# Attention output stored without its normalisation and scaled at the first expert layer's input; the products with V grouped, the near scores put between them

## The reference

```python
q_rot, k_rot = rotate(q), rotate(k)                       # q, k, v: (4, 8, 576, 64), float32
scores = (1 / sqrt(64)) * q_rot @ k_rot.T
scores = scores - max(scores, axis=-1)
attn = exp(scores)
attn = attn / (sum(attn, axis=-1) + 1e-09)
x = attn @ v                                              # rearranged to (2304 tokens, 512)
h = x @ w_in1;  x = (h - tanh(h)) @ w_out1                # w_in (512, 2048), w_out (2048, 512)
h = x @ w_in2;  out = (h * sigmoid(1.702 * h)) @ w_out2
```

## Time and profile before

| | |
|---|---|
| runs, median | 1148.81 us |
| profiled execution | 1147.27 us, of which the span is 1145.5 us |
| PE busy | 1104.1 us, 96% |
| DVE busy | 552.4 us, 48% |
| ACT busy | 425.7 us, 37% |
| POOL busy | 57.1 us, 5% |
| R of head 0, R of head 31 | at 23.05 us, at 325.15 us |
| first expert matmul | at 337.05 us |

### The profile page before, as it was taken

How to read it: one execution, slowest core, us unless ns; L and a number is a source line. 1 busy time by engine, 2 the same in 40 slices (tenths; PEclk the granted TensorE clock), 3 DMA queues, 4 the chain that set the end, 5 groups by cost and what they waited for, 6 DMA issues and landing times.

```text
span 1145.5 us, 15078 instructions
## 1 busy us (share of the span) xinstructions
PE 1104.1 (96%) x5952; PEld 1017.8 (89%) x5952; DVE 552.4 (48%) x879; ACT 425.7 (37%) x747; POOL 57.1 (5%) x62
## 2 busy tenths in 40 slices
PE   2999998999999999999999999999999999999998
PEld 1888877787789999999999999999999999999997
DVE  7888887888736433232233333455232322323222
ACT  2555554555544423222222323445232222323222
POOL 3011111102111000000000000000000000000000
PEclk9999999999999999999999999999999999999999
DMA  6355557566315300000000100062000000000000
GB/s 182 95 158 127 155 154 201 136 169 166 87 61 178 102 28 29 28 28 11 19 28 28 29 28 28 1 193 83 28 28 28 28 1 28 28 28 1 28 1 28
DMA packets 78854, 79.85 MB, mean 70 GB/s; under 512 B 30144, under 2 KB 55744, under 8 KB 78784
## 3 DMA queue, kind: packets, MB, share of 16 engines
q1 hardware_dynamic: 78784, 78.89, 24.1%
HBM read 55.12 MB, written 14.23 MB: 61 GB/s over the span
## 4 chain that ended last, share of the span: by engine, by line
PE 89%; DVE 7%; SPq 1%; DMA 1%; POOL 1%; issue 1%; ACT 0%; POOLq 0%; DVEq 0%; ACTq 0%
PE PS L485 35%; PE PS L503 17%; PE PS L500 17%; PE PS L449 10%; PE PS L414 3%; PE PS L431 3%; PE PS L437 3%; DVE neg_max L667 2%; DVE q_max L684 1%; DVE k_hl L679 1%; DVE q_max L674 1%; DMA turned_k<-k_dram 1%; DVE raw_q L662 0%; DVE w_parts L697 0%; DVE raw_q L660 0%
## 5 line engine op out<-in xcount | busy, mean ns | idle before, releaser
L485 PE MATMUL PS<-x_hi,w_parts 128*128 128x384 f32 x1536 | 423.1, 336 | 0.0
L742 DVE TENSOR_TENSOR g_raw<-PS,act_t 128x384 f32<-128x384 f32 x192 | 107.0, 557 | 400.2 <-ACT act_t L610 202.1
L485 PEld LDWEIGHTS PS<-x_hi,w_parts 128*128 128x128 f32 x1536 | 280.5, 188 | 4.3
L485 PE MATMUL PS<-x_lo,w_parts 128*128 128x384 f32 x768 | 257.2, 335 | 0.0
L500 PE MATMUL PS<-g_hi,w_parts 128*128 128x384 f32 x768 | 210.3, 334 | 0.8 <-DVE g_lo L747 0.8
L503 PE MATMUL PS<-w_parts,g_hi 128*128 128x512 f32 x576 | 195.1, 393 | 1.0 <-DVE y_sb L756 0.8
L449 PE MATMUL PS<-probs,v_one 128*128 128x288 f32 x640 | 183.4, 409 | 0.3 <-ACT pv_sb L545 0.3
L747 DVE TENSOR_TENSOR g_lo<-g_raw,g_hi 128x384 fp32r<-128x384 f32 x192 | 107.7, 561 | 113.6 <-ACT g_hi L617 113.6
L537 ACT ACTIVATE probs<-PS 128x576 f32<-128x576 f32 x160 | 104.0, 650 | 129.6 <-PE PS L437 126.3
L485 PEld LDWEIGHTS PS<-x_lo,w_parts 128*128 128x128 f32 x768 | 144.2, 188 | 4.2
L617 ACT ACTIVATE g_hi<-g_raw 128x384 fp32r<-128x384 f32 x192 | 100.8, 525 | 122.9 <-DVE g_raw L742 119.7
(11 more groups left out here) (51 smaller groups left out, 741.3 us busy)
## 6 DMA issues: line engine op xcount, KB each, us to landing
x_raw<-x_scratch SPq DMA_DIRECT2D x12, 768.0 KB, 4.5
raw_w<-moe_w_in_dram SPq DMA_DIRECT2D x32, 256.0 KB, 3.1
raw_w<-moe_w_out_dram SPq DMA_DIRECT2D x32, 256.0 KB, 3.3
raw_k<-k_dram SPq DMA_DIRECT2D x16, 288.0 KB, 3.5
turned_k<-k_dram SPq DMA_DIRECT2D x64, 72.0 KB, 3.2
raw_q<-q_dram SPq DMA_DIRECT2D x16, 288.0 KB, 3.8
turned_q<-q_dram SPq DMA_DIRECT2D x64, 72.0 KB, 3.5
k_one<-k_hl SPq DMA_DIRECT2D x32, 144.0 KB, 2.4
```

The lines of the kernel that those rows point to most:

```text
L485: last = nc.tensor.matmul(h_banks[j % 2], w_parts[j][:, w, c * P:(c + 1) * P], x[par][:, c, :], start=(c == 0 and w == 0 and x is x_hi), s ...
L742: nc.vector.tensor_tensor(g_raw[:, j % 2, :], h_banks[j % 2], act_t[:, j % 2, :], ALU.subtract if m == 0 else ALU.mult).then_inc(g_done, 1)
```

## The change

Three edits, made together.

1. `pv_sb` goes to `x_scratch` as it is, one DMA a head, from SP right behind that head's sums. The inverses go to `inv_scratch`, laid out as x is. `load_x` of the first layer fetches, beside x, the inverses of the unit in two DMAs that repeat each row over 64 partitions, into the new tile `inverses`. DVE multiplies x by them (`scale_x`, four instructions of 128x384 a unit) ahead of `cut_x`, and ACT's part of `cut_x` waits for each. `spread_inverse`, `normalise` and POOL's `tile_mask` are gone. In iterations 17 and 19, ACT's part of `cut_x` is now behind the exponential of tile 4 in place of tile 2.
2. `place_maxima` is moved from DVE to ACT: five copies of 5x128 instead of one DVE instruction of 5x640, each with a column of the identity as its per-partition scale, behind the exponential of tile 2.
3. The order of PE and with it `RING`: PV comes in groups of two, one and two, and the near scores of tiles 1 to 4 stand singly or in a pair around them.

```diff
-PV_LAG = 2
+NEAR_BEFORE = {0: (1,), 1: (4,)}
+NEAR_AFTER = {0: (2, 3)}
...
             def store_inverse(pair):
+                row, col = pair % PAIRS_PER_BATCH, pair // PAIRS_PER_BATCH * SEQ
...
-            def spread_inverse(pair):
...
-            def store_x(pair):
...
+            def store_x(h):
+                pair, a = h // 2, h % 2
+                row, col = pair % PAIRS_PER_BATCH * P + a * HD, pair // PAIRS_PER_BATCH * SEQ
+                sp.wait_ge(pv_copied, h + 1)
+                sp.dma_start(x_scratch[0][row:row + HD, col:col + SEQ], pv_sb[h % 4][own(a), :]).then_inc(x_stored[h % 4], 16)
...  load_x
+                if m == 0:
+                    for j in range(2):
+                        sp.wait_ge(inv_out[j], 16 * batches * PAIRS_PER_BATCH // 2)
+                    if u:
+                        sp.wait_ge(x_scaled, u * KC)
+                    for a in range(2):
+                        rows = inv_scratch.rearrange("c a n -> a c n")[a:a + 1, :, u * UNIT:(u + 1) * UNIT]
+                        sp.dma_start(inverses[own(a), :, :], rows.broadcast_to([HD, KC, UNIT])).then_inc(inverses_in, 16)
...  POOL
-            nc.gpsimd.memset(tile_mask, 0.0).then_inc(pool_chain, 1)
...
-            def normalise(pair):
...
-                for a in range(2):
-                    last = nc.gpsimd.tensor_tensor(x_out[par][own(a), :], pv_sb[(2 * pair + a) % 4][own(a), :],
-                                                   inv_wide[par][own(a), :], ALU.mult)
...  PE
                     if now:
                         scores(h, t)
-                    if now and g >= 0:
-                        probs_v(g)
-                    if ahead and t < 2:
-                        near_scores(h + 1, 2 * t + 1)
-                        near_scores(h + 1, 2 * t + 2)
+                        if ahead:
+                            for i in NEAR_BEFORE.get(t, ()):
+                                near_scores(h + 1, i)
...
+                    if t == 0 and h >= 1:
+                        probs_v(h * TILES - 3)
+                        probs_v(h * TILES - 2)
+                    if t == 1 and h >= 1:
+                        probs_v(h * TILES - 1)
+                    if t == 3 and now:
+                        probs_v(h * TILES)
+                        probs_v(h * TILES + 1)
+                    if now and ahead:
+                        for i in NEAR_AFTER.get(t, ()):
+                            near_scores(h + 1, i)
...  ACT
+            def place_maxima(h):
+
+                act.wait_ge(r_ready, h + 1)
+                for t in range(TILES):
+                    last = nc.scalar.activation(q_max[h % 4][max_rows(h % 2), t * P:(t + 1) * P],
+                                                slot_of("R", h)[0:TILES, 0, 0:P], ACT.Copy, scale=ident[0:TILES, t:t + 1])
+                last.then_inc(row_done, 1)
...
-                    if t == 2 and h in early_x:
+                    if t == 2 and 0 <= h + 1 < NHEADS:
+                        place_maxima(h + 1)
+                    if t == 4 and h in early_x:
                         cut_x(0, 0, 0, early_x[h])
...  DVE
-            def place_maxima(h):
...
+            def scale_x(u, chunks=range(KC)):
+                dve.wait_ge(x_loaded, u * 16 + 16)
+                dve.wait_ge(inverses_in, u * 32 + 32)
+                for c in chunks:
+                    nc.vector.tensor_tensor(x_raw[:, c, :], x_raw[:, c, :], inverses[:, c, :], ALU.mult).then_inc(x_scaled, 1)
```

More of the change, by code:

```diff
@@ L53, in ring_order @@
                 order.append(("S", h, t))
-            if ahead and t < 2:
-                order += [("M", h + 1, 2 * t + 1), ("M", h + 1, 2 * t + 2)]
-            if ahead and t == 2:
-                order.append(("R", h + 1, 0))
+            if ahead:
+                order += [("M", h + 1, i) for i in (NEAR_BEFORE if now else {}).get(t, ())]
+                order += [("M", h + 1, i) for i in NEAR_AFTER.get(t, ()) if now]
+                if not now and t == 0:
+                    order += [("M", h + 1, i) for i in range(1, TILES)]
+                if t == 2:
+                    order.append(("R", h + 1, 0))
         if h + 2 < NHEADS:
@@ L96, in program @@
         y_sb = sb("y_sb", [P, KC, BANK])
+        inverses = sb("inverses", [P, KC, UNIT])
         w_parts = [sb(f"w_parts{j}", [P, 4, BANK], F32R) for j in range(APART)]
@@ L115, in program @@
         sums = [sb(f"sums{j}", [P, 2 * SEQ // P], stack=one_stack) for j in range(2)]
-        inv_wide = [sb(f"inv_wide{j}", [P, SEQ], stack=one_stack) for j in range(2)]
-        x_out = [sb(f"x_out{j}", [P, SEQ], stack=one_stack) for j in range(2)]
         one_stack.close()
@@ L150, in program @@
         inv_done = sem("inv_done")
-        inv_out = sem("inv_out")
-        inv_in = [sem(f"inv_in{j}") for j in range(2)]
-        norm_done = sem("norm_done")
-        x_stored = [sem(f"x_stored{j}") for j in range(2)]
+        inv_out = [sem(f"inv_out{j}") for j in range(2)]
+        inverses_in = sem("inverses_in")
+        x_scaled = sem("x_scaled")
+        x_stored = [sem(f"x_stored{j}") for j in range(4)]
         raw_w_in = [sem(f"raw_w_in{j}") for j in range(STAGING)]
@@ L258, in load_x @@
                     batches = ((u + 1) * UNIT - 1) // SEQ + 1
-                    for j in range(2):
+                    for j in range(4):
                         sp.wait_ge(x_stored[j], 16 * batches * PAIRS_PER_BATCH // 2)
@@ L290, in _ @@
                     load("q", q_d, pair + 2)
[L291 to L294 removed]
                 if h >= 1:
                     fetch_sums(h - 1)
+                    store_x(h - 1)
                 if h >= 0 and h % 2 == 0 and h // 2 + 1 < PAIRS:
@@ L457, in _ @@
                 for t in range(TILES):
-                    g = h * TILES + t - PV_LAG
                     if now:
                         scores(h, t)
-                    if now and g >= 0:
-                        probs_v(g)
-                    if ahead and t < 2:
-                        near_scores(h + 1, 2 * t + 1)
-                        near_scores(h + 1, 2 * t + 2)
+                        if ahead:
+                            for i in NEAR_BEFORE.get(t, ()):
+                                near_scores(h + 1, i)
+                    elif ahead and t == 0:
+                        for i in range(1, TILES):
+                            near_scores(h + 1, i)
[9 more added lines that the diff above has]
+                        for i in NEAR_AFTER.get(t, ()):
+                            near_scores(h + 1, i)
                     if ahead and t == 2:
@@ L567, in cut_weights @@
                 if m == 0 and c == 13:
-                    act.wait_ge(x_stored[0], 16 * (PAIRS // 2))
-                    act.wait_ge(x_stored[1], 16 * (PAIRS // 2))
+                    for j in range(4):
+                        act.wait_ge(x_stored[j], 16 * (NHEADS // 4))
                 if m:
@@ L707, in _ @@
                 dve.wait_ge(cleared, j + 1)
-                last = nc.vector.memset(k_one[j][max_rows(j % 2), :].bitcast(F32), 1.0)
+                last = nc.vector.memset(k_one[j][max_rows(j % 2), 0:SEQ].bitcast(F32), 1.0)
             last.then_inc(pads_set, 1)
@@ L723, in _ @@
                     rope("kq"[h % 2], h // 2 + 2)
-                if 0 <= h + 1 < NHEADS:
-                    place_maxima(h + 1)
                 if -2 <= h < 0:
```

50 lines of the change are left out of this document (11 added, 39 removed).

## The result

The changed kernel takes 1156.2 us (median of four runs, 1155.49 to 1158.01), the kernel before 1148.66 us beside it; the ratio is 1.0068 with an interval of 1.005 to 1.0085. It is slower, by 7.5 us where 4.9 were forecast. Its profiled execution took 1155.49 us with a span of 1153.7, 8.2 above the span before.

The account below looks back on a forecast made before the run. PE was taken to set the pace in the heads, with DVE close behind. Heads +6.1, front -2.5 and first expert unit +1.3 gave +4.9 us, so 1153.7 us was forecast, with a range of 1137 to 1163.

Parts of the forecast that it names:

- The step it rests on: In each head, moving place_maxima (0.8 us) off DVE leaves the chain to M0's maximum unmoved, since ACT sets it.
- The first rival: Near scores' waits in the heads don't bind and DVE's relief shows: 1138, or 1134 without old short waits; chance 0.27.
- the narrow forecast: Whole kernel slower by 2.5 to 9 us, at 1151 to 1158 us; chance 0.40.
- Heads, by their terms: R to R: even 9.96 for 9.24, odd 9.46 for 8.96; iterations 17 and 19 10.9, four with weights 10.3.
- So the 18.5 us go altogether: Time above plain heads, in iterations 14 to 27, vanishes once POOL stops multiplying and SP stops waiting for it: -18.5 us.
- the extra DMAs ... I count 0: Loading x a head earlier and 0.8 MB of inverses a unit costs 0, as they start where PE has slack.
- the reason given: In the heads, POOL's multiplying and DVE's two-input instructions lock each other out, and SP waits for POOL; both end.
- The heads' 6.1: Net change of the heads: +10.8 even, +4.5 odd, +3.9 with x, +5.4 with weights, -18.5 gone, so +6.1 us.
- Placing on ACT: Five ACT copies a head take 0.28 each at 0.20 spacing, 1.1 us, leaving the last exponential not late.
- The rival "dear": Placing on ACT makes heads late by 0.2 us and more, its queue being shared: 1160 us; chance 0.15.
- Front and experts: All starts 1.4 earlier, first R at 21.6, front and end together -2.5 us; first expert unit +1.3 us.
- The clock: Rival: clock falls again in the heads as PE idles in each, some 1.7 us a fall, three make 1159; chance 0.05.

Follow-up runs that it names:

- placing on DVE: Changed kernel with place_maxima back on DVE, so edits 1 and 3 without edit 2; 1151.6 us, ratio 1.0031 to the kernel before.
- store alone: Kernel before with edit 1 only: unnormalised store, DVE scaling x, placing on DVE and PE's order as before; 1146.23 us, ratio 0.9987.
- high part first: store alone with ACT's queries_hi moved ahead of the last exponential; 1142.07 us, ratio 0.9952 to the kernel before.
- pair at the end: store alone with two PV together between the last S and M0, near scores as before; 1143.68 us, ratio 0.9969 to the kernel before.

## Why the prediction was right, and where its sizes were off

**The step it rests on held.** "Taking `place_maxima` off DVE does not move this chain, since ACT sets it": with DVE placing, `queries_lo` still waits 1.58 us for ACT; with ACT's part moved forward, the head gets shorter, by 0.22 us in even heads. The first rival (the relief of DVE shows, 1134 to 1138) needed M4 and S1 not to wait. They wait, in even heads and in odd ones. The time lies in the narrow forecast of 1151 to 1158 us, 2.5 above its centre.

**Heads, by their terms.** Even 9.96 forecast, 9.94 measured; odd 9.46 and 9.54. The 0.08 in the odd heads is the placing: the last exponential stands at E+0.24 to 0.3 in place of 0.20, and M0's maximum at E+2.20 (E+2.13 with placing on DVE). Heads with x 10.9 and 11.03, with weights 10.3 and 10.67. By the run without edit 2 (9.46) the whole of the extra 1.2 in these four comes from placing and cut of weights in one stretch of ACT's queue. The increases over the old lengths are 10.5 (fifteen even heads, at 0.70), 5.2, 4.1 and 6.8, together 26.6, where 10.8, 4.5, 3.9 and 5.4, together 24.6, were forecast.

**The term that was mis-sized: "So the 18.5 us go altogether", with "the extra DMAs ... I count 0".** Interval 15 took 11.32 us before and 11.76 after, 1.8 above its even neighbours. The wait before was DVE's, behind POOL, and went; a new one took its place. SP issues x and inverses ahead of the next copy of `q_hh`, which is issued 1.8 us later for it and lands 8.1 us behind its issue in place of 3.3; with x loaded in iteration 24 the interval takes 9.95. The prediction had asked only whether PE has slack where the loads start, and not what stands behind them in the same queues. The 1.8 us `<- issue` of the kernel before is such a wait as well: the copy issued at 182.06 lands 4.4 later, and the matmul starts at 186.51. So part of the 18.5 hung on the DMA queues and not on POOL.

The rest did go, but not for the reason given, and that its size came out is in part luck: store alone, which has the whole of that reason, took 8.7 of the 18.5 and laid 5.1 beside them, and the remainder went with the other two edits (interval 17: 15.41 before, 11.05 with edit 1, 10.71 with 1 and 3, 9.96 with all). For edit 2 the traces show how. With placing on DVE, PE waits 1.23 us in interval 17 for `place_maxima`, and DVE is late with it because its rotation waited 1.73 us for the DMA of `turned_k`. With placing on ACT the slot of R comes free without DVE, and no wait for `q_max` is left among PE's. That gain of edit 2 stands nowhere in the prediction. The heads' 6.1 with 1.8 for interval 15, 1.4 for the weights and 0.7 for the odd heads make 10.0, against 9.8 measured.

The Trainium skill (SBUF — State Buffer, Who interferes with whom) is borne out on the lock itself, by 843 against 750 ns for the same DVE instruction. Thirteen of them gained 1.2 us of DVE time; how much of that lay on PE's path is not shown.

**Placing on ACT.** Five took 1.34 us, not 1.1; the trace after, all of them (lowest, median, highest ns):

```profile
L544 ACT ACTIVATE q_max<-PS,ident x160: 340/342/357, 22.3 to 333.4; 5x128 fp32r<-5x128 f32 x160
```

That is 342 ns each at a spacing of 250. The estimate by the Trainium skill (ScalarE: Activation LUTs, What ACT_TABLE_LOAD costs) was 1.6 for five; the measurement lies between it and mine. The rival "dear" was false in the new order (0.08 us an odd head, 1.2 in four others) and true in the old one. By the ratios, with edit 1 in place, edit 2 costs 9.4 us (0.82%) in the old order and 4.3 (0.37%, after against placing on DVE) in the new one; edit 3 costs 5.1 (0.44%) with the placing on DVE and nothing that can be told from noise with it on ACT. The two edits are not additive. An even head takes 9.25 with neither, 9.83 with edit 2, 9.87 with edit 3 and 9.94 with both: the heads lengthen by 0.58 and 0.62 alone and by 0.69 together, as if each drew on the same slack.

**Front and experts.** First R at 21.88 (21.6 forecast), the front and the end together -2.9 where -2.5 was forecast. But not all started 1.4 us earlier: the first matmul did not move, 17.46 in both traces, because it waits for the DMA of `q_hh`. What went is a wait of 1.06 us behind it for DVE's maxima. In the other traces that first matmul stands anywhere from 16.67 to 19.15, and first R, in the four other kernels that have no mask from POOL, at 21.57 (twice), 22.62 and 23.35; so that it came within 0.3 of the forecast is in part luck. The multiplication of x in the first expert unit:

```profile
383.53 1.96 DVE L702 TENSOR_TENSOR x_raw<-x_raw,inverses 128x384 f32<-128x384 f32 x4
```

1.96 us against 1.9 taken. PE's waits for `g_lo` in the experts grew by 1.0, and the experts by 1.25 (1.3 forecast).

**The clock** fell nowhere in the heads of the profiled execution after, so that rival was false, and the two falls of before are part of what was given back. The mean clocks of whole executions agree: three of four after read 1.0 and one 0.998, while of fourteen of before one read 1.0.

**What stays open.** Why the clock fell behind some waits and not behind others and how the 8.7 us of edit 1 divide between POOL and SP.

## What to carry to other kernels

Before an operation is moved from a busy engine to an idle one, find whose result the busy one waits for next: if it is the idle one's, the move shortens nothing, and what it adds to the idle one's queue can lengthen the path. Price an order by the whole walk from one fixed point of the loop to the next, with every queue, since two edits can draw on the same slack. A DMA that is added delays those issued behind it twice, by its place in the issuing queue and by its bytes, which lengthen their way to landing; price both against the time at which the first reader comes.

## What the runs showed of the hardware that was not expected

An ACT copy of only 5 partitions by 128 columns from PSUM, with a scale for each partition, took 342 ns at 250 ns of spacing, against 644 ns for an exponential of 128x576: small ones are not cheap.

The same SBUF to SBUF copy of `q_hh` took 2.2 to 3.7 us from issue to landing between 40 and 150 us of the kernel after, and 8.1 us behind the loads of x and inverses, while the DMA engines moved 249 GB/s.

The granted clock fell to half for 3.4 us behind some of PE's waits and not behind others as long. In the kernel after, behind the wait of 2.31 us:

```profile
172.00:177.00 5.00, 4.78 (x27) 4.15 (x28) 3.27 (x7) 1.15 (x2) 0.00 (x0) 1.00 0.39 76
```

In high part first, behind one of 2.09:

```profile
217.00:227.00 10.00, 7.91 (x38) 6.79 (x38) 7.44 (x11) 3.54 (x6) 0.00 (x0) 0.83 0.19 41
```

The first reads 1.00, the second 0.83. In their profiled executions, five of the six other kernels with the new order had no fall. Executions of one kernel differ too: in nine of pair at the end the mean clock went from 0.995 (1146.72 us) to 1.0 (1142.57 us).
